# Softmax reciprocals spread by a transpose, attention batches written out, and a reordered prologue

## What is computed

```
s_pos = np.maximum(s, 0.0)
cum = np.cumsum(s_pos, axis=-1)
bias = -(cum[:, :, :, None] - cum[:, :, None, :])
scores = np.where(causal, -1000000000.0, scores + np.minimum(bias, 0.0))
scores = scores - np.max(scores, axis=-1, keepdims=True)
attn = np.exp(scores)
attn = attn / (np.sum(attn, axis=-1, keepdims=True) + 1e-09)
return np.matmul(attn, v)
```

## Time and profile before

| | us |
|---|---|
| median of 3 runs | 1106.84 (1105.74 to 1106.98) |
| the profiled execution | 1111.58 |
| its span, first to last instruction | 1109.8 |
| PE matmuls busy | 1080.0 |
| DVE busy | 444.0 |
| ACT busy | 418.7 |
| POOL busy | 168.4 |
| mean granted TensorE clock | 0.990 |

### The profile page before, as it was taken

The page is one execution under the profiler, slowest core; times in us unless marked ns, Lnnn a source line. Parts: engine busy times, 40 slices in busy tenths (PEclk is TensorE's granted clock), DMA queues, the critical chain, the costliest instruction groups (busy, mean ns, idle before and its releaser), DMA issues.

```text
span 1109.8 us, 19419 instructions
## 1 busy us (share of the span) xinstructions
PE 1080.0 (97%) x6836; PEld 998.6 (90%) x6836; DVE 444.0 (40%) x1214; ACT 418.7 (38%) x1030; POOL 168.4 (15%) x178
## 2 busy tenths in 40 slices
PE   4999999899999999999999999999999999999998
PEld 3888787789999999999999999999999999899997
DVE  6677677554432321321322333433223232332322
ACT  4676667664422232222222233433223232332322
POOL 4777777730000000000000000000000000000000
PEclk9999999899999999999999999999999999999999
DMA  5444455213200000000000122310000000000000
GB/s 187 150 150 150 154 157 152 85 32 96 67 1 1 1 0 0 0 0 0 0 0 0 29 76 77 95 29 29 1 1 29 0 28 0 0 28 0 28 0 28
DMA packets 48452, 51.66 MB, mean 47 GB/s; under 512 B 2990, under 2 KB 38830, under 8 KB 48394
## 3 DMA queue, kind: packets, MB, share of 16 engines
q1 hardware_dynamic: 48394, 50.94, 14.8%
HBM read 41.63 MB, written 4.87 MB: 42 GB/s over the span
## 4 chain that ended last, share of the span: by engine, by line
PE 95%; issue 1%; DVE 1%; DMA 1%; POOL 1%; ACT 1%; SPq 0%; ACTq 0%; DVEq 0%; POOLq 0%
PE HP L954 15%; PE HP L956 15%; PE HP L955 15%; PE YP L955 11%; PE YP L956 11%; PE YP L954 11%; PE TP L892 5%; PE OP L908 5%; PE SC L879 4%; PE OP L920 2%; PE SC L880 2%; DMA Qraw<-in_qT 0%; ACT PT L451 0%; DMA QO<-QA 0%; PE MP L927 0%
## 5 line engine op out<-in xcount | busy, mean ns | idle before, releaser
L954 PE MATMUL HP<-XS,WA 128*128 128x384 f32 x576 | 194.6, 338 | 0.3 <-ACT AC L518 0.3
L956 PE MATMUL HP<-XS,WA 128*128 128x384 f32 x576 | 193.0, 335 | 0.0
L955 PE MATMUL HP<-XS,WA 128*128 128x384 f32 x576 | 192.7, 335 | 0.0
L760 DVE TENSOR_TENSOR AC<-AC,HP 128x384 f32<-128x384 f32 (+2 forms) x78 | 40.3, 523 | 294.1 <-PE HP L956 294.1
L811 DVE TENSOR_TENSOR AC<-HP,AC 128x384 f32<-128x384 f32 (+1 forms) x108 | 54.3, 512 | 216.3 <-ACT AC L580 216.3
L580 ACT ACTIVATE AC<-HP 128x384 f32<-128x384 f32 x96 | 47.2, 492 | 215.7 <-PE HP L956 215.2
L954 PEld LDWEIGHTS HP<-XS,WA 128*128 128x128 f32 x576 | 108.2, 188 | 3.0 <-issue 0.5
L955 PEld LDWEIGHTS HP<-XS,WA 128*128 128x128 f32 x576 | 108.2, 188 | 2.4
L956 PEld LDWEIGHTS HP<-XS,WA 128*128 128x128 f32 x576 | 108.1, 188 | 0.0
L518 ACT ACTIVATE AC<-HP 128x384 f32<-128x384 f32 x72 | 35.4, 492 | 178.3 <-PE HP L956 178.3
L954 PE MATMUL YP<-HS,WX 128*128 128x384 f32 (+2 forms) x312 | 102.1, 327 | 0.5 <-DVE HS L766 0.5
(11 more groups left out here) (109 smaller groups left out, 2029.3 us busy)
## 6 DMA issues: line engine op xcount, KB each, us to landing
X<-in_w SPq DMA_DIRECT2D x52, 256.0 KB, 3.3
Kraw<-in_kT SPq DMA_DIRECT2D x16, 576.0 KB, 4.8
Qraw<-in_qT SPq DMA_DIRECT2D x16, 576.0 KB, 5.6
out_rows<-OS SPq DMA_DIRECT2D x18, 256.0 KB, 2.2
QO<-QA SPq DMA_DIRECT2D x15, 288.0 KB, 3.3
Vt<-in_v SPq DMA_DIRECT2D x16, 256.0 KB, 3.1
WRAW<-in_w SPq DMA_DIRECT2D x16, 256.0 KB, 2.8
Vt<-in_v SPq DMA_DIRECT2D x16, 32.0 KB, 2.1
```

What stands on the lines that cost most here:

```text
L760: dve.tensor_tensor(AC[:, m % 2, cols], AC[:, m % 2, cols], HP[:, 1, cols], ALU.mult).then_inc(prod_done if part is None else prod_part, 1)
L954: pe.matmul(dst, w(0), x(0), start=start, stop=False)
L955: pe.matmul(dst, w(0), x(1), start=False, stop=False)
L956: return pe.matmul(dst, w(1), x(0), start=False, stop=stop)
```

## The change

1. Spread: after the reciprocal, DVE waits for it and copies it into a new tile `RW`, 64 times over for each head, in one instruction. PE transposes `RW` with one instruction in place of the two plain matmuls. The tile `RR` no longer needs its preset.
2. The loops over batches 1 and 2 are gone from the lists of all five engines; all four batches are written out.
3. In `prepare`, POOL no longer waits for the transfer into QO; PE still does.
4. In the prologue, SP issues the loads of pair 1 ahead of the KD rows. The constants of QO and Vt are set by POOL instead of DVE, `onesm` and `eps` too (behind pair 0's QA), and DVE sets the padding of PR after the running sum.

```diff
@@ sync
             load_qk(0, 0, 0)
+            load_qk(0, 1, 1)
             for row, part in enumerate((cum_hi, cum_lo)):
                 sp.wait_ge(cum_step, 4 + row)
...
-            load_qk(0, 1, 1)
...
@@ gpsimd
+            pool.wait_ge(consts, 2)
+            for j in range(2):
+                pool.memset(QO[D:D + 2, j].bitcast(F32), 1.0).then_inc(padded, 1)
+            for j in range(2):
+                pool.wait_ge(padded, j + 2)
+                pool.memset(Vt[0:P - PAD, j, 0, :], 0.0).then_inc(padded, 1)
+            pool.wait_ge(padded, 4)
...
-                pool.wait_ge(qo_in[j], 16 * (2 * b + p // 2 + j))
...
-            batch(0)
-            with pool.Fori(1, B - 1) as b:
-                batch(b)
-            batch(B - 1, last=True)
+            pool.memset(onesm[:], 1.0 / DM).then_inc(onesm_set, 1)
+            pool.memset(eps[:], RMS_EPS).then_inc(onesm_set, 1)
+            for b in range(B):
+                batch(b, last=(b == B - 1))
@@ vector
-            for j in range(4):
-                dve.memset(PR[:, j, :, 0:PAD], 0.0).then_inc(padded, 1)
-            dve.memset(RR[:], 1.0).then_inc(padded, 1)
...
-            for j in range(2):
-                dve.memset(QO[D:D + 2, j].bitcast(F32), 1.0).then_inc(padded, 1)
-            for j in range(2):
-                dve.memset(Vt[0:P - PAD, j, 0, :], 0.0).then_inc(padded, 1)
...
-            dve.memset(onesm[:], 1.0 / DM).then_inc(onesm_set, 1)
-            dve.memset(eps[:], RMS_EPS).then_inc(onesm_set, 1)
+            for j in range(4):
+                dve.memset(PR[:, j, :, 0:PAD], 0.0).then_inc(pr_padded, 1)
...
                 dve.reciprocal(RR[0:z, n % 4], RE[0:z, n % 4]).then_inc(recip_done, 1)
+                dve.wait_ge(recip_done, b * STEPS + n + 1)
+                wait(dve, spread_mm, b * STEPS + n - 1)
+                dve.nop(nofuse=True)
+                dve.tensor_copy(RW[0:z, n % 2], RR[0:z, n % 4].rearrange("p (h o) -> p h o", o=1)
+                                .broadcast_to([z, 2, D])).then_inc(wide_done, 1)
@@ tensor
-                pe.wait_ge(recip_done, b * STEPS + n + 1)
+                pe.wait_ge(wide_done, b * STEPS + n + 1)
                 wait(pe, o_evac, b * STEPS + n - 1)
                 pe.nop(nofuse=True)
-                for hh in range(2):
-                    last = pe.matmul(OP[hh * D:(hh + 1) * D, n % 2, 0:z],
-                                     RR[:, n % 4, hh:hh + 1].broadcast_to([P, D]), ident[:, 0:z],
-                                     start=True, stop=True)
-                last.then_inc(spread_mm, 1)
+                pe.transpose(OP[:, n % 2, 0:z],
+                             RW[0:z, n % 2].rearrange("p h d -> p (h d)"), ident[0:z, 0:z]).then_inc(spread_mm, 1)
```

More of the change, by code:

```diff
@@ L37 @@
 R_LAG = 2
+ALL = B * STEPS
 SQ_STEPS, MS_STEP, ROOT_STEP = (0, 1, 2, QB), 8, 2 * QB
@@ L146, in build @@
         RR = sb("RR", [P, 4, 2], F32)
+        RW = sb("RW", [P, 2, 2, D], F32)
         RB = sb("RB", [P, 2, P], F32)
@@ L208, in build @@
         const_step = sem("const_step"); consts = sem("consts"); cum_step = sem("cum_step")
-        padded = sem("padded"); eps_set = sem("eps_set")
+        padded = sem("padded"); pr_padded = sem("pr_padded"); eps_set = sem("eps_set")
         k_hi = sem("k_hi"); q_hi = sem("q_hi"); k_lo = sem("k_lo"); q_lo = sem("q_lo")
         scores_done = sem("scores_done"); mins_done = sem("mins_done"); exp_done = sem("exp_done")
-        eps_done = sem("eps_done"); recip_done = sem("recip_done")
+        eps_done = sem("eps_done"); recip_done = sem("recip_done"); wide_done = sem("wide_done")
         spread_mm = sem("spread_mm"); spread_done = sem("spread_done")
@@ L293, in _ @@
             sp.wait_ge(cum_out, 32)
[L295 to L299, removed]
+            for k in range(B * PAIRS):
+                at, after = divmod(k + 1, PAIRS), divmod(k + 2, PAIRS)
+                if k + 1 < B * PAIRS:
+                    wait(sp, scores_done, 2 * QB * k)
                     load_decay(*at)
-                    sp.wait_ge(q_hi, 2 * (b * PAIRS + p + 2))
+                    sp.wait_ge(q_hi, 2 * (k + 2))
                     load_qo(*at)
-                if not last or p + 2 < PAIRS:
-                    if isinstance(b, int) and b * PAIRS + p == 0:
+                if k + 2 < B * PAIRS:
+                    if k == 0:
                         sp.wait_ge(qo_first, 2)
@@ L308, in load_ahead @@
                     else:
[L309 to L316, removed]
-                    load_weights(*after)
[L319 to L325, removed]
+                        sp.wait_ge(k_lo, 2 * k)
+                        sp.wait_ge(q_lo, 2 * k)
+                    load_qk(*after, k % 2)
+                if k + 1 < B * PAIRS:
+                    wait(sp, pv_done, QB * k)
+                    load_v(*at, (k + 1) % 2)
+                if k + 2 < B * PAIRS:
+                    sp.wait_ge(w_lo, k + 1)
+                    load_weights(*after)
             for k, (src, _, i, sem_free, count) in enumerate(loads):
@@ L502, in _ @@
                 act.activation(QO[0:D, 0, hh], Qraw[0:D, 0, hh], ACT.Copy).then_inc(qo_first, 1)
[L503 to L506, removed]
+            for b in range(B):
+                batch(b, first=(b == 0), last=(b == B - 1))
             for n in range(R_LAG + 1):
@@ L855, in _ @@
             pe.wait_ge(consts, 2)
-            pe.wait_ge(padded, 9)
+            pe.wait_ge(padded, 4)
+            pe.wait_ge(pr_padded, 4)
             def scores(b, n, hh):
```

## The result

The changed kernel takes 1153.49 us (median of 4 runs, 1152.12 to 1157.75) against 1106.43 (4 runs, 1105.74 to 1106.98) for the kernel before on the same chip: ratio 1.0433, 95% interval 1.0416 to 1.0449. It is 47 us slower. I had forecast slower, but by 7 us, and the measured time lies outside my range.

The account below looks back on a forecast made before the run. PE, busy 97%, bounds the kernel, with DVE close to holding it up. Start -6.2, pairs 2 to 12 +11.8, last three +1.5: together +7 on the median 1106.84, giving 1114 us, range 1094 to 1130.

Parts of the forecast that it names:

- The direction and the mechanism: Attention stage: slower, because DVE's wide copy waits until POOL's current instruction is over and PE waits behind DVE.
- the race for the u4 copy: Step u4 of a pair: wide copy races POOL's first long instruction; losing costs +1.4 us, half entered, +0.7.
- the copy in u1: Step u1 of a pair: wide copy lies among POOL's 1.41 us instructions; mean wait 0.7, cost +0.62 us.
- the lost race: Every pair's u4 copy comes behind POOL's first long instruction: pairs of 15.3 us, against 13.9 if won.
- Rival 3: Attention pairs: race lost and PE's clock falls; 1123 us from pairs alone, 1130 with half at low clock; chance 0.15.
- the price of the loop's turn: Loop's turn before the change: PE's 1.51 us gap came with clock 0.90 and cost 1.6 us beyond the gap.
- The row against it: Profile row of a pair with an extra DVE add: PE idled 0.40 us and the clock stayed full.
- POOL's wait for QO: POOL's split work: removing the wait is worth nothing to PE; only POOL's period falls from 13 to 10.9 us.
- The spread's own saving: PE in each attention pair: one transpose replacing two matmuls per step saves 0.71 us, 11.4 in 16 pairs.
- the pair's formula, 12.35 + 3c: Attention pair length in us without the lock, c being DVE's cost per step, 0.18 to 0.25.
- Prologue and unrolling: Start: first matmul at 10.5 us, pair 1's wait for POOL gone; loop's turn like other pairs, -3.2 us.
- my rival without a wait: Attention stage: the copy doesn't meet POOL, takes 0.15 to 0.22 us; pairs 13.1, total 1096 us; chance 0.26.

Follow-up runs that it names:

- e4: The changed kernel with extra, never-read matmuls (8 and 14 per pair) filling PE's two long waits; 1135.2 us.
- e6: The changed kernel with DVE's wide copy still written but unused, PE keeping the old plain matmuls; 1147.2 us.
- e9: The changed kernel with each of POOL's four long subtractions of a pair cut into two halves; 1117.4 us.
- e1: The changed kernel without the spread: no wide copy, the old pair of matmuls, all other parts kept; 1096.8 us.
- e8: The changed kernel with POOL's wait for the QO transfer put back; 1120.6 us.
- e5: The changed kernel without the wide copy, PE transposing a buffer of ones, so the result lacks the division by row sums; 1090.2 us.
- e3: The changed kernel with DVE's wide copy written as a tensor_reduce over one element; 1108.4 us.
- e10: The kernel before with only its batch loops written out; 1104.3 us.
- e12: Repeat of the changed kernel without the spread (old matmuls, no wide copy), in five rounds; 1097.1 us.

## Why the prediction was wrong, step by step

The two profiled spans differ by 43.0 us. Cut as in the prediction's sum: start to pair 2 -0.9 (40.69 for 41.61; predicted -6.2), pairs 2 to 12 +38.4 (186.5 for 148.1; predicted +11.8), the rest +5.5 (predicted +1.5). So the miss of 36 us is 5 at the start, 27 in the middle and 4 at the end.

**The direction and the mechanism were right.** The copy meets POOL, waits for the whole instruction, and ends 0.08 behind it (I had said 0.07). The first matmul came at 10.46 for 10.5. The order of transpose, gap, values is as I drew it (57.95, then 58.15).

**The step that failed: the price of the race for the u4 copy.** I took it as a draw and entered half of its 1.4, and a mean wait of 0.7 for the copy in u1. It isn't a draw. POOL's instructions and DVE's copy both follow from the scores of u4, and their distance hardly moves: the copy comes 0.08 to 0.09 us after POOL's start, on the losing side, in every pair from 40.69 to 207.43 but the one of 14.47 us (the same in most pairs of e4, e6 and e9). The wait couples the engines further: DVE is let go when POOL's instruction ends, so its next copy falls at the same point of POOL's third one (0.13 us into it). Both copies are held for nearly a whole instruction (1.34 to 1.40). The first of PE's stalls came as priced (0.87 for 0.9), the second took 1.59 where my terms leave some 1.3. The pair is 15.6 us, near the 15.3 that I had given to the lost race. (My own terms add up to 15.13 for it, and to 14.43 for the forecast, not 14.5; I had rounded up on the way.) With the stalls filled, in e4, pairs 2 to 12 take 172.2 us for my 159.9: 12 us are this step, 2.5 of them the spread's smaller saving (below).

**The second term: the clock.** Rival 3 had the right mechanism and half the pairs, but the price of the loop's turn, 1.6 us a fall, on stalls of 1 to 1.4 us. A fall costs 2.95 (18.55 - 15.6), at a clock of 0.82 over the pair and not 0.90. Cut finer, the windows tell why. The first row is of the change, the second of before at the loop's turn, the third of e6:

```profile
63.56:70.39 6.83, 6.83 (x46) 5.22 (x45) 2.38 (x11) 2.12 (x9) 2.40 (x3) 0.50 0.01 2
```

```profile
124.64:128.05 3.41, 3.41 (x20) 2.92 (x16) 2.24 (x9) 1.51 (x7) 1.49 (x3) 0.50 0.75 188
```

```profile
126.47:129.89 3.42, 3.01 (x23) 2.38 (x23) 0.96 (x4) 0.82 (x3) 3.06 (x3) 0.50 0.04 15
```

In each PE runs at half its clock (1.2 GHz). In the change it does so for 6.8 us, from 0.4 us behind its stall of 1.59 on; at the turn, from which I took the price, for 3.4. The falls are 18 us in all (e4), 14 of them in pairs 2 to 12 (186.5 - 172.2). I gave that rival 0.15 and let it end at 1130. The row against it (a gap of 0.40 left the clock full) spoke only of gaps a quarter as long.

**The start.** Pair 0 took 12.37 us for my 10.4 and pair 1 17.86 for 14.5. Pair 1 has held copies and a fall like the later ones. In pair 0 PE's instructions keep their long durations for longer than in e1. The same scores in the change and, below, in e1:

```profile
20.72 0.44 PE L875 MATMUL SC<-KD,QO 66*128 66x288 f32 x1
```

```profile
19.35 0.30 PE L871 MATMUL SC<-KD,QO 66*128 66x288 f32 x1
```

What makes the difference in pair 0 wasn't tested.

**POOL's wait for QO.** "Worth nothing there" was argued from PE, which never stands idle for it. I even wrote that POOL's period falls, and then didn't ask where in DVE's order its instructions would land. e8 prices this at 33 us. e8 stands 24 us above e1, the change 57. Without such a copy on DVE (e1) the missing wait shows no harm.

**The spread's own saving** was 0.48 a pair, not 0.71 (e5 against e1), and the pair's formula, 12.35 + 3c, gives 13.2 for e3 where 13.59 was measured; 0.23 of the 0.39 is this term.

**Prologue and unrolling** were right, and hidden: e1 reaches pair 2 at 34.68, 6.9 earlier than before (my terms give 34.0 with a pair of 13.1). In the change pair 1 is slow at a clock of 0.81 again, for DVE and no longer for POOL. e10 puts the unrolling at -2.8 (predicted -3.2), and e12 against e10 leaves 7.2 us for the prologue and the wait for QO together; the two were not run apart.

Taken together, with the parts read from different runs, the change is: prologue, wait and unrolling -10, the transpose -7 (e5 against e1), the unblocked length of the copy on DVE +18 (e3 against e5), its waits +27 and the clock +18 (together e3 to the change): +46, where +47 was measured.

**Open.** Why the clock falls in every second pair of the change, and with the old matmuls (e6) for half as long in each, isn't known; the stalls are alike in pairs with and without a fall. Nor is the length of a stall enough to tell. In the second pair from the end PE is idle for 1.68 us in e1 (to 199.53) and in e5 (to 194.63) alike; in e1 the clock is halved for 3.4 us from 199.98 on, in e5 it stays full. The stalls of 1.2 to 1.3 us in e8 left it full as well. The 4 us at the end were not taken apart.

## What to carry to other kernels

Before you put a small SBUF-to-SBUF copy on VectorE, look at what GpSimd is doing at that moment: the copy can cost as much as GpSimd's longest instruction, not its own 0.23 us. If it must be there, another form (a reduce) or another engine (ScalarE) avoids the wait, and shorter GpSimd instructions bound it. When two engines are released by the same event, work out their order to 0.1 us instead of averaging over it, and price the stalls of TensorE with the clock: here a stall of 1.59 us was followed in every second pair by a fall that cost 2.95.

## What the runs showed of the hardware

- VectorE's copy of 128 floats with a source of two elements read 64 times each takes 0.227 us free, and ends 0.08 us behind GpSimd's instruction when held up. Its free length alone didn't tell that it would wait: my rival without a wait allowed up to 0.22. The reduce of the same size takes 0.284, 0.057 more. VectorE's copies out of PSUM take 0.13 us more for each 128 elements (0.42, 0.55 and 0.68 us for 256, 384 and 512), and 0.057 is near half of that. As an estimate from these rows, and if their fixed parts are alike, the free copy moves two elements in the time in which the reduce moves one.
- Held up by GpSimd, the copy took up to 1.46 us; the form as a reduce was never held up in 80 (0.289 at most). A copy that began 0.02 us ahead of GpSimd's instruction lengthened that one by 0.07 us (e8).
- Two stalls of 0.87 and 1.59 us in a pair came with 6.8 us at half clock in every second pair. With the stalls filled it stayed full (e4), and with one stall of 1.0 us (e9) or of up to 1.3 us (e8) in a pair it did until the last pair.
- A wait on GpSimd for a transfer that its next instructions don't need moved the time of the kernel by 33 us, by the phase of one engine alone.
